# The low parts of the attention scores as two 64-row matmuls, one per half of the keys

## The chip, the cores and the metric

One core of one Trainium2 chip. The metric is the device time of one execution in microseconds (us), the median of several runs. PE is TensorE (matmuls; its weight loads are listed as PEld), DVE is VectorE, ACT is ScalarE, POOL is GpSimd, SP is SyncE, which issues nearly all DMAs.

## What is computed

Attention over 4 batches x 8 heads (32 heads here, sequence 576, head dimension 64) with an additive position bias, and two feed-forward layers behind it:

```python
scores = scale * np.matmul(q, k.transpose(0, 1, 3, 2)) + bias
attn = softmax(scores)                 # over the keys, denominator + 1e-9
x = np.matmul(attn, v)                 # heads side by side: 2304 tokens x 512
r = np.maximum(x @ w_in, 0.0)
x = (s * r * r + b) @ w_out            # 512 -> 2048 -> 512
h = x @ w_in2
out = (h - np.tanh(h)) @ w_out2        # 512 -> 2048 -> 512
```

The bias is the product of a two-layer network of log distances, one 576 x 576 map for each of the 8 heads.

## The kernel before

Products that need more than one matmul pass's precision are made from high and low parts: `x` is rounded to a shorter float (`high`), and `x - high` is `low`. q and k arrive from memory twice, stacked: partitions 0 to 63 and 64 to 127 hold the same 64 x 576 values (`q_raw`, `k_raw`). For q, ACT writes `q2 = round(q_raw * lower)` (L199), where `lower` is 0 in the upper 64 partitions and 1 in the lower ones, and POOL writes `q2 = q_raw - q2` (L209). So partitions 0 to 63 of `q2` hold q's high parts and 64 to 127 its low parts. For k, POOL writes `k2h = round(k_raw)` (L204) and `k2l = k_raw - k2h` (L213), both over all 128 partitions. One matmul of `q2` with `k2h` gives high*high + low*high, one with `k2l` gives high*low + low*low.

A head is five steps (t = 0 to 4, `NT` = 5) of 128 rows of scores each, the last padded. Step g = 5 n + t does on PE (`pe_step`): the scores of head n, tile t (`pe_score`, L576 to 582: two halves of 288 keys, each in a PSUM bank of its own, a matmul with `k2h` and one with `k2l` per half, 4 in all); the product of earlier probabilities with v (`pe_value`, L556 and 559, for heads 0 to 9; `pe_value_planes`, L541 and 544, from head 10 on); and for heads 0 to 9 the transposition of the probabilities (`pe_turn`, L592). DVE adds the bias and takes the minimum (L764), ACT does the exponential (L640). From head 10 on the probabilities are written as two 16-bit planes (ACT L628, DVE L743), turned by a DMA (SP L807), and POOL casts the high plane to `pth` (L686) for the value matmul L541 of the step after.

Order on the engines is the order of the program text; semaphores tie them together. POOL in a step (`pool_step`): at t = 0 the rounding and low part of k of the next head, then the cast for a value matmul (from head 12 on), at t = 1 the scaling of x (L714, every other head, heads 0 to 9) and q's low part of the next head, at t = 3 the parts of v. ACT rounds q of the next head at the end of its t = 1. SP (`sp_step`) issues in each step the next head's bias tile (L219), then a plane's turning; at t = 1 the load of v, at t = 2 that of k and at t = 4 that of q two heads ahead (L817 to 821). Each raw buffer is single: `load_q` waits for `q_lo_done`, `load_k` for `k_lo_done`.

Up to 70 us the position bias is built (`*_biases`; PE multiplies in four 32-column tiles side by side, L424). Then steps run alone (`STEPS_AT[:FIRST]`, 49 steps, until about 181 us). From there the 5 x 64 feed-forward blocks run (`pe_block`, 12 matmuls each, L903 to 905; their low weights come from POOL, L860, three blocks ahead, behind ACT's high weights, L853), and the other steps are put between them at the places of the list `PLACES`: behind every second block in parts, behind every block in others. Heads 10 and on lie there, until about 745 us.

`o_tmp` holds the lower half of a head's output for a moment (ACT L645 writes it, DVE L781 reads it).

Of the kernel before, what the change touches and what calls it, by code (L numbers as in the profile page):

```python
# [5 lines left out]
F32 = mybir.dt.float32  # L6
# [6 lines left out]
P = 128  # L13
# [18 lines left out]
def build(nc, qt, kt, vt, net, w2s, psi, lam, lam_rows, sb, w1, w2, w3, w4, out):  # L32
# [53 lines left out]
    with ExitStack() as ctx:  # L86
# [11 lines left out]
        v_raw = tile("v_raw", [P, 2 * NT - 1, D])  # L98
        q2 = tile("q2", [P, 2, NT * P], F32R)
        k2h = tile("k2h", [P, 2, S], F32R)  # L100
        k2l = tile("k2l", [P, 2, S], F32R)
        bias_t = tile("bias_t", [P, NT, S])

        zero_done = sem("zero_done")
# [21 lines left out]
        v_hi_done = sem("v_hi_done")  # L126
        q_lo_done = sem("q_lo_done")
        k_lo_done = sem("k_lo_done")
        v_lo_done = sem("v_lo_done")
        s_done = sem("s_done")  # L130
        min_done = sem("min_done")
# [74 lines left out]
        def pool_low_q(pool, n):  # L206
            pool.wait_ge(q_hi_done, n + 1)
            both = q2[:, n % 2, 0:S]
            pool.tensor_tensor(both, q_raw[:], both.bitcast(F32), ALU.subtract).then_inc(q_lo_done, 1)  # L209

        def pool_low_k(pool, n):
            pool.wait_ge(k_hi_done, n + 1)
            pool.tensor_tensor(k2l[:, n % 2, :], k_raw[:], k2h[:, n % 2, :].bitcast(F32), ALU.subtract)\  # L213
                .then_inc(k_lo_done, 1)

        def sp_bias(sp, n, t):
            R = ROWS[t]
# [6 lines left out]
        with nc.sbuf_tensor("ptl", [P, 2, S], F32R) as ptl:  # L224
            pass
        planes = tile("planes", [P, 2, 2 * S], F16)
        o_tmp = tile("o_tmp", [D, 2, HALF])
        neg_max = tile("neg_max", [P, NT])
        den = tile("den", [P, 2, NT])
        den_e = tile("den_e", [P, NT])  # L230
# [98 lines left out]
        def act_biases(act):  # L329
            act.dma_start(net_c, net).then_inc(net_loaded, DMA)  # L330
            act.dma_start(lam_c, lam).then_inc(psi_loaded, DMA)
            act.wait_ge(table_done, 2)

            def hidden(pack):
                need(act, hid_used, pack - HIDS + 1)
                n = reach(pack)
                for at in range(VEC, PACK):
                    step = pack * PACK + at
                    mm = act.activation(hid[:, pack % HIDS, at, 0:n], psi_w[:, 0:n], ACT.Relu,  # L339
                                        bias=knee[:, step:step + 1])  # L340
                mm.then_inc(hid_act, 1)

            hidden(0)
            act.wait_ge(table_done, 4)
            for pack in range(PACKS):
                if pack + 1 < PACKS:
                    hidden(pack + 1)
                back, ahead = backward(pack), forward(pack)
                act.wait_ge(hid_used, pack + 1)
                if pack >= RES_BUFS:  # L350
                    act.wait_ge(stage_stored[pack % RES_BUFS], pack // RES_BUFS * DMA)
                for acc, lo, hi in chunks(pack):
                    hi = min(hi, ahead)
                    if lo < hi:
                        dst = stage[:, pack % RES_BUFS, back + lo:back + hi]
                        mm = act.activation(dst, acc[:, 0:hi - lo], ACT.Copy,  # L356
                                            scale=row_scale[:, pack:pack + 1])
                mm.then_inc(ahead_done, 1)
                if pack == LATE:
                    act.wait_ge(q_clear, 2)  # L360
                    act.wait_ge(lower_done, 2)
                    act_round_q(act, 0)

        def pool_biases(pool):
            pool.memset(ident[:], 0.0).then_inc(zero_done, 1)
            pool.memset(bias_t[:, NT - 1, :], 0.0).then_inc(bias_clear, 1)
            for par in range(2):
                pool.memset(q2[:, par, S:NT * P].bitcast(F32), 0.0).then_inc(q_clear, 1)
            pool.wait_ge(zero_done, 1)
            pool.affine_select(out=ident[:], in_=ident[:], compare_op=ALU.not_equal, fill=1.0, base=0,  # L370
                               pattern=[[-1, P]], channel_multiplier=1).then_inc(ident_done, 1)
            pool_round_k(pool, 0)
            pool_low_k(pool, 0)
            pool_low_q(pool, 0)

        def dve_biases(dve):
# [145 lines left out]
        def cast(g):  # L522

            return g - NT - 2 if FIRST_PLANE <= g - NT - 2 < TILES else None
# [38 lines left out]
        def pe_score(pe, n, t):  # L563
            if t == 0:
                pe.wait_ge(q_lo_done, n + 1)
                pe.wait_ge(k_lo_done, n + 1)
            if n == 0:
                need(pe, min_done, t - 1)
                pe.wait_ge(back_done, PACKS - 2 if t == 0 else PACKS)
            elif n <= TURNED:  # L570
                pe.wait_ge(min_done, n * NT + t)
            else:
                if n == TURNED + 1 and t == 0:
                    pe.wait_ge(pt_lo_done, FIRST_PLANE)
                pe.wait_ge(p_lo_done, n * NT + t - FIRST_PLANE - 1)
            for half in range(2):  # L576
                cols = slice(half * HALF, (half + 1) * HALF)
                acc = score_bank(n, t)[:, half, 0:HALF]
                lhs = q2[:, n % 2, P * t:P * (t + 1)]
                pe.matmul(acc, lhs, k2h[:, n % 2, cols], start=True, stop=False)  # L580
                mm = pe.matmul(acc, lhs, k2l[:, n % 2, cols], start=False, stop=True)  # L581
            mm.then_inc(s_done, 1)

        def pe_turn(pe, i, alone):
# [46 lines left out]
        def act_step(act, g, alone, between=None):  # L631
            n, t = divmod(g, NT)
            i, j = turned(g), valued(g)

            def exponential():
                if t == 0:
                    need(act, den_done, min(n - 1, TURNED))
                act.wait_ge(min_done, g + 1)
                p = score_home(n, t)
                act.activation(p, p, ACT.Exp, scale=-1.0, bias=neg_max[:, t:t + 1],  # L640
                               accum_out=den[:, n % 2, t:t + 1]).then_inc(exp_done, 1)

            if j is not None and j % NT == NT - 1:
                act.wait_ge(pv_done, j + 1)
                act.activation(o_tmp[:], ps_o[D:P, :, 0:HALF], ACT.Copy, scale=1.0 if j < FIRST_PLANE else PLANE)\  # L645
                    .then_inc(o_low_done, 1)
            f = planes_of(g)
            if f is not None:
                act_plane(act, f)
            if scoring(n) and alone and t == NT - 1:  # L650
                exponential()
            if i is not None:
                R = ROWS[i % NT]
                act.wait_ge(pt_done, i + 1)
                need(act, pv_done, i - 1)
                act.activation(pth[0:R, slot(i), :], turn_bank(i, alone)[0:R, 0:S], ACT.Copy)\
                    .then_inc(pt_hi_done, 1)
            if n < TURNED and between:
                between()
            if scoring(n) and not (alone and t == NT - 1):  # L660
                exponential()
            if n >= TURNED and between:
                between()
            if TURNED <= n < BH:
                act.wait_ge(exp_done, g + 1)
                act.activation(sum_n[:, t:t + 1], den[:, n % 2, t:t + 1], ACT.Copy, scale=PLANE, bias=1e-9 * PLANE)\
                    .then_inc(sum_done, 1)
            if t == 0 and turning(n):
                v = n - 1
                need(act, inv_done, v)  # L670
                act.wait_ge(exp_done, (v + 1) * NT)
                act.activation(den_e[:], den[:, v % 2, :], ACT.Copy, bias=1e-9).then_inc(den_done, 1)
            if t == 1 and n + 1 < BH:
                act_round_q(act, n + 1)

        def pool_step(pool, g):
            n, t = divmod(g, NT)
            if t == 0 and n + 1 < BH:
                pool_round_k(pool, n + 1)
                pool_low_k(pool, n + 1)  # L680
            i = cast(g)
            if i is not None:
                if i % NT == 0:
# [63 lines left out]
        def dve_step(dve, g, alone, between=None):  # L747
# [29 lines left out]
            if j is not None and j % NT == NT - 1:  # L777
                h = j // NT
                dve.wait_ge(o_low_done, h + 1)
                dst = x_slice(h, slice(h % 2 * D, (h % 2 + 1) * D))  # L780
                dve.scalar_tensor_tensor(out=halves(dst), in0=ps_o[0:D, :, 0:HALF],  # L781
                                         scalar=1.0 if h < TURNED else PLANE, in1=o_tmp[:],
                                         op0=ALU.mult, op1=ALU.add).then_inc(o_done, 1)
            if between:
                between()
# [1 line left out]
        def sp_step(sp, g):  # L787
# [29 lines left out]
                load_v(sp, n)  # L817
            if t == 2 and n + 2 < BH:
                load_k(sp, n + 2)
            if t == 4 and n + 2 < BH:  # L820
                load_q(sp, n + 2)

        def raw_block(b):
# [230 lines left out]
        def _(pe):  # L1054
            pe_biases(pe)
            pe.wait_ge(ident_done, 1)
            pe.wait_ge(q_clear, 2)
            for g in STEPS_AT[:FIRST]:
                pe_step(pe, g, True)
            pe.wait_ge(pt_lo_done, turned(FIRST - 1))  # L1060
# [68 lines left out]
```

## Time and profile before

| | |
|---|---|
| median of 3 runs | 1100.48 us (1098.94 to 1100.62) |
| profiled execution, its own time | 1100.58 us |
| its span from first to last instruction | 1098.8 us |
| granted TensorE clock, mean | 0.995 |
| PE busy | 1050.3 us (96%), 5668 matmuls |
| DVE, ACT, POOL busy | 617.6 us, 732.3 us, 680.9 us |

Durations in the profile are of single instructions. Matmuls are pipelined: one is listed as 0.29 to 0.38 us long, while the next may start 0.13 or 0.21 us after it, so what PE's stream costs is read from start to start. A time in square brackets behind an instruction is how long its engine sat idle before it and what released it.

### The profile page before, as it was taken

To read this page: it belongs to the slowest core of one execution; us is meant where nothing else is said; L and a number is where in the kernel's file an instruction comes from. 1 tells how busy PE (TensorE), PEld (TensorE's weight loads), DVE (VectorE), ACT (ScalarE), POOL (GpSimd) and SP (SyncE) were. 2 spreads that over 40 slices of the span, in tenths; PEclk is the share of its full clock that TensorE was granted. 3 is DMA by queue.
4 is the path that set the end of the run, shared out by engine and by line. 5 is a ranking of instruction groups with operands and counts; after the bars stand their busy time and mean duration, and the time that the engine had idled before them with its cause. 6 is when DMAs were issued, how large, how long until landed. Compare 5 with 4: busy or idle time off the path is not lost.

```text
span 1098.8 us, 16840 instructions
## 1 busy us (share of the span) xinstructions
PE 1050.3 (96%) x5668; PEld 912.9 (83%) x5668; DVE 617.6 (56%) x1120; ACT 732.3 (67%) x1477; POOL 680.9 (62%) x656
## 2 busy tenths in 40 slices
PE   4669999999999999999999999999999999999998
PEld 1148889888888888888888888888888888999998
DVE  5968877745775476468646754771350451440640
ACT  8968887866877687678767776873562563553652
POOL 1046675677778677777786777765554555455453
PEclk9989999999999999999999999999999999999999
DMA  4678876799779778987896799764323233332331
GB/s 166 242 247 260 278 228 173 190 245 239 193 213 263 211 196 216 258 216 203 237 275 167 193 256 263 174 161 130 112 98 115 96 107 131 106 129 101 97 122 64
DMA packets 185482, 202.51 MB, mean 184 GB/s; under 512 B 125954, under 2 KB 128692, under 8 KB 185396
## 3 DMA queue, kind: packets, MB, share of 16 engines
q1 hardware_dynamic: 185108, 201.35, 65.5%
q8 instruction: 46, 0.75, 0.3%
q14 instruction: 40, 0.33, 0.1%
q10 hardware_dynamic: 288, 0.07, 0.0%
HBM read 156.55 MB, written 15.64 MB: 157 GB/s over the span
## 4 chain that ended last, share of the span: by engine, by line
PE 71%; ACT 11%; issue 7%; POOL 5%; DVE 4%; DMA 2%; SPq 0%; DVEq 0%; ACTq 0%; POOLq 0%
PE ps_f L903 20%; PE ps_f L905 20%; PE ps_f L904 20%; ACT x_raw L339 3%; POOL wl L860 2%; PE ps_o L541 2%; DVE g_buf L963 2%; PE ps_s L580 2%; PE ps_s L581 2%; ACT gh L916 2%; PE ps_o L544 2%; ACT stage L356 2%; PE ps_o L556 1%; POOL pth L686 1%; ACT planes L628 1%
## 5 line engine op out<-in xcount | busy, mean ns | idle before, releaser
L860 POOL TENSOR_TENSOR wl<-w_raw,wh 128x512 fp32r<-128x512 f32 x318 | 417.0, 1317 | 285.2 <-ACT wh L853 284.7
L903 PE MATMUL ps_f<-gh,wh 128*128 128x464 f32 (+1 forms) x640 | 243.3, 380 | 1.6 <-DVE g_buf L963 1.6
L903 PE MATMUL ps_f<-xh,wh 128*128 128x464 f32 (+1 forms) x640 | 240.6, 376 | 0.6 <-DVE ptl L732 0.6
L904 PE MATMUL ps_f<-gl,wh 128*128 128x464 f32 (+1 forms) x640 | 238.1, 372 | 0.0
L905 PE MATMUL ps_f<-gh,wl 128*128 128x464 f32 (+1 forms) x640 | 237.9, 372 | 0.0
L905 PE MATMUL ps_f<-xh,wl 128*128 128x464 f32 (+1 forms) x640 | 237.5, 371 | 0.0
L904 PE MATMUL ps_f<-xl,wh 128*128 128x464 f32 (+1 forms) x640 | 237.2, 371 | 0.0
L853 ACT ACTIVATE wh<-w_raw 128x512 fp32r<-128x512 f32 x318 | 196.4, 623 | 49.1 <-PE ps_f L905 48.6
L903 PEld LDWEIGHTS ps_f<-gh,wh 128*128 128x128 f32 x640 | 121.3, 190 | 14.9 <-DVE g_buf L963 2.8
L903 PEld LDWEIGHTS ps_f<-xh,wh 128*128 128x128 f32 x640 | 120.5, 188 | 13.3 <-DVE ptl L732 0.8
L905 PEld LDWEIGHTS ps_f<-gh,wl 128*128 128x128 f32 x640 | 120.6, 188 | 13.0
L905 PEld LDWEIGHTS ps_f<-xh,wl 128*128 128x128 f32 x640 | 120.2, 188 | 13.4
L904 PEld LDWEIGHTS ps_f<-xl,wh 128*128 128x128 f32 x640 | 120.2, 188 | 12.7
L904 PEld LDWEIGHTS ps_f<-gl,wh 128*128 128x128 f32 x640 | 120.7, 189 | 11.8
L926 ACT ACTIVATE r_buf<-ps_f 128x464 f32<-128x464 f32 (+1 forms) x160 | 87.9, 550 | 59.2 <-PE ps_f L905 58.3
L954 DVE TENSOR_TENSOR gl<-g_buf,gh 128x464 fp32r<-128x464 f32 (+1 forms) x80 | 81.3, 1016 | 47.5 <-ACT gh L920 47.5
L951 DVE SCALAR_TENSOR_TENSOR gl<-g_buf,sb_c,gh 128x464 fp32r<-128x464 f32 (+1 forms) x80 | 73.9, 924 | 52.9 <-ACT gh L916 52.9
L963 DVE SCALAR_TENSOR_TENSOR g_buf<-ps_f,sb_c,r_buf 128x464 f32<-128x464 f32 (+1 forms) x80 | 55.4, 693 | 41.6 <-ACT r_buf L926 40.2
L686 POOL CAST pth<-p_t 128x576 fp32r<-128x576 f16 x110 | 77.5, 704 | 0.0
L209 POOL TENSOR_TENSOR q<-q_raw,q 128x576 fp32r<-128x576 f32 x32 | 45.9, 1434 | 46.1 <-ACT q L199 46.1
L580 PE MATMUL ps_s<-k2h,q 128*128 128x288 f32 x210 | 65.4, 326 | 5.7 <-DVE neg_max L764 5.7
L916 ACT ACTIVATE gh<-g_buf,sb_c 128x464 fp32r<-128x464 f32 (+1 forms) x80 | 54.3, 678 | 20.9 <-DVE g_buf L963 20.9
(124 smaller groups left out, 1693.0 us busy)
## 6 DMA issues: line engine op xcount, KB each, us to landing
w_raw<-in_w_out SPq DMA_DIRECT2D x80, 512.0 KB, 3.6
w_raw<-in_w_in SPq DMA_DIRECT2D x79, 512.0 KB, 3.5
bias_t<-bias_flat SPq DMA_DIRECT2D x128, 288.0 KB, 4.0
bias_flat<-stage SPq DMA_DIRECT2D x36, 295.5 KB, 2.2
k_raw<-in_kt SPq DMA_DIRECT2D x32, 288.0 KB, 4.0
q_raw<-in_qt SPq DMA_DIRECT2D x32, 288.0 KB, 3.3
v_raw<-in_vt SPq DMA_DIRECT2D x32, 288.0 KB, 3.2
bias_t<-bias_flat SPq DMA_DIRECT2D x32, 144.0 KB, 4.1
```

What stands on the lines that cost most here:

```text
L580: pe.matmul(acc, lhs, k2h[:, n % 2, cols], start=True, stop=False)
L686: pool.tensor_copy(pth[:, slot(i), :], turned_planes(i // NT)[:, i % NT, :]).then_inc(block_cast, 1)
L853: act.activation(wh[:, b % RING, :, :], raw_block(b), ACT.Copy)\
L860: pool.tensor_tensor(wl[:, b % RING, :, :], raw_block(b), wh[:, b % RING, :, :].bitcast(F32), ALU.subtract).then_inc(w_lo_done, 1)
L903: pe.matmul(acc, hi, rhs_h[:, k0 + kk, 0:T], start=(first and kk == 0), stop=False)
L904: pe.matmul(acc, hi, rhs_l[:, k0 + kk, 0:T], start=False, stop=False)
L905: mm = pe.matmul(acc, lo, rhs_h[:, k0 + kk, 0:T], start=False, stop=(last and kk == 3))
L916: act.activation(gh[:, j, 0:T], g_buf[:, n % 2, 0:T], ACT.Identity, bias=sb_c[:, 1:2])\
L926: act.activation(r_buf[:, n % 2, 0:T], acc, (ACT.Relu, ACT.Tanh)[l]).then_inc(r_done, 1)
L951: dve.scalar_tensor_tensor(out=gl[:, j, 0:T], in0=g_buf[:, n % 2, 0:T], scalar=sb_c[:, 1:2], in1=hi, op0=ALU.add, op1=ALU.subtract).then_i ...
L954: dve.tensor_tensor(gl[:, j, 0:T], g_buf[:, n % 2, 0:T], hi, ALU.subtract)\
L963: dve.scalar_tensor_tensor(out=g_buf[:, n % 2, 0:T], in0=acc, scalar=sb_c[:, 0:1], in1=r, op0=ALU.mult, op1=ALU.mult).then_inc(g_done, 1)
```

## The change

`k2l` keeps for each half of the partitions only one half of the keys: partitions 0 to 63 hold k's low parts for keys 0 to 287, 64 to 127 those for keys 288 to 575. POOL writes it with two subtractions of 64 partitions x 288, the second after the first has ended. q's high parts are needed in the lower partitions too: POOL copies `q_raw` there into a new tile with rounding (`q_even`, `q_odd` by head), at t = 0 behind k's low part, and goes on when the copy has ended. In `pe_score` the two matmuls with `k2h` come first, then two of 64 rows: q's high parts from partitions 0 to 63 with the left half of k's low parts into the first bank, and from partitions 64 to 127 with the right half into the second. The product of the two low parts is no longer computed. `o_tmp` uses partitions 0 to 63 of the place where `q_even` uses 64 to 127. The load of q is issued at t = 3 in place of t = 4.

```diff
-        k2l = tile("k2l", [P, 2, S], F32R)
+        k2l = tile("k2l", [P, 2, HALF], F32R)
+        q_odd = tile("q_odd", [P, NT * P], F32R)
+        with nc.sbuf_tensor("o_tmp", [P, 2, HALF], F32) as o_tmp:
+            pass
+        q_even = tile("q_even", [P, NT * P], F32R)
...
         def pool_low_k(pool, n):
             pool.wait_ge(k_hi_done, n + 1)
-            pool.tensor_tensor(k2l[:, n % 2, :], k_raw[:], k2h[:, n % 2, :].bitcast(F32), ALU.subtract)\
-                .then_inc(k_lo_done, 1)
+            pool.tensor_tensor(k2l[0:D, n % 2, :], k_raw[0:D, 0:HALF], k2h[0:D, n % 2, 0:HALF].bitcast(F32),
+                               ALU.subtract).then_inc(k_left_done, 1)
+            pool.wait_ge(k_left_done, n + 1)
+            pool.tensor_tensor(k2l[D:P, n % 2, :], k_raw[D:P, HALF:S], k2h[D:P, n % 2, HALF:S].bitcast(F32),
+                               ALU.subtract).then_inc(k_lo_done, 1)
+
+        def q_below(n):
+
+            return q_odd if n % 2 else q_even
+
+        def pool_round_q(pool, n):
+            pool.wait_ge(q_loaded, (n + 1) * DMA)
+            pool.wait_ge(k_lo_done, n + 1)
+            pool.tensor_copy(q_below(n)[D:P, 0:S], q_raw[D:P, :]).then_inc(q_below_done, 1)
+            pool.wait_ge(q_below_done, n + 1)
...
             for par in range(2):
                 pool.memset(q2[:, par, S:NT * P].bitcast(F32), 0.0).then_inc(q_clear, 1)
+                pool.memset(q_below(par)[:, S:NT * P].bitcast(F32), 0.0).then_inc(q_clear, 1)
...
             pool_round_k(pool, 0)
             pool_low_k(pool, 0)
+            pool_round_q(pool, 0)
             pool_low_q(pool, 0)
...
                 pe.matmul(acc, lhs, k2h[:, n % 2, cols], start=True, stop=False)
-                mm = pe.matmul(acc, lhs, k2l[:, n % 2, cols], start=False, stop=True)
+            for half, high in ((0, q2[0:D, n % 2, P * t:P * (t + 1)]), (1, q_below(n)[D:P, P * t:P * (t + 1)])):
+                acc = score_bank(n, t)[:, half, 0:HALF]
+                mm = pe.matmul(acc, high, k2l[half * D:(half + 1) * D, n % 2, :], start=False, stop=True)
             mm.then_inc(s_done, 1)
...
             if t == 0 and n + 1 < BH:
                 pool_round_k(pool, n + 1)
                 pool_low_k(pool, n + 1)
+                pool_round_q(pool, n + 1)
...
-            if t == 4 and n + 2 < BH:
+            if t == 3 and n + 2 < BH:
                 load_q(sp, n + 2)
```

## Rows read from the trace of the kernel before

**Rows 1.** Busy time by stretch: stretch, its length, busy us of each engine (instructions), clock.

```profile
70.00:181.00 111.00, 103.93 (x681) 92.81 (x682) 87.09 (x184) 90.29 (x193) 69.31 (x69) 0.97 0.78 244
181.00:745.00 564.00, 556.65 (x2916) 490.45 (x2915) 356.33 (x665) 413.65 (x867) 418.34 (x426) 1.00 0.85 217
```

**Rows 2.** PE in order of time, mixed stretch: start us, duration us, engine, line, operation.

```profile
400.35 0.37 PE L905 MATMUL ps_f<-xh,wl 128*128 128x464 f32 x1
400.56 0.30 PE L580 MATMUL ps_t<-k2h,q 128*128 128x288 f32 x1
400.69 0.29 PE L581 MATMUL ps_t<-k2l,q 128*128 128x288 f32 x1
```

**Rows 3.** The matmuls and weight loads of L581 alone, by stretch.

```profile
70.00:181.00 111.00, 27.10 (x94) 18.63 (x94) 0.97 0.78 244
181.00:745.00 564.00, 60.18 (x216) 40.59 (x216) 1.00 0.85 217
```

**Rows 4.** PE and its loads in order of time, full array to 64 columns.

```profile
129.92 0.29 PE L559 MATMUL ps_o<-ptl,vhl 128*128 128x288 f32 x1
...
129.93 0.57 PEld L592 LDWEIGHTS ps_t<-ident,p_t 128*64 128x64 f32 x5
...
130.05 0.71 PE L592 MATMUL ps_t<-ident,p_t 128*64 128x128 f32 x5
```

**Rows 5.** PE in order of time where 32-column tiles end and scores begin.

```profile
61.85 1.18 PE L424 MATMUL ps_o<-x_raw,y 128*32 128x288 f32 x16 [0.37 <-ACT x_raw L339]
...
62.58 0.45 PE L424 MATMUL ps_o<-x_raw,y 128*32 128x288 f32 x4
...
62.96 0.40 PE L580 MATMUL ps_s<-k2h,q 128*128 128x288 f32 x1
63.20 0.30 PE L581 MATMUL ps_s<-k2l,q 128*128 128x288 f32 x1
```

**Rows 6.** POOL by line, 181 to 745 us: shapes, count | busy us, mean ns | idle before.

```profile
L860 POOL TENSOR_TENSOR wl<-w_raw,wh 128x512 fp32r<-128x512 f32 x173 | 228.3, 1322 | 115.0 <-ACT wh L853 114.7
...
L213 POOL TENSOR_TENSOR k2l<-k_raw,k2h 128x576 fp32r<-128x576 f32 x20 | 29.0, 1450 | 1.6
L705 POOL TENSOR_TENSOR vhl<-v_raw,vhl 128x320 fp32r<-128x320 f32 x22 | 20.5, 932 | 0.0
```

**Rows 7.** POOL and PE in order of time at a head's first step.

```profile
332.00 0.67 POOL L204 CAST k2h<-k_raw 128x576 fp32r<-128x576 f32 x1
...
332.75 1.41 POOL L213 TENSOR_TENSOR k2l<-k_raw,k2h 128x576 fp32r<-128x576 f32 x1
...
334.12 1.07 POOL L686 CAST pth<-p_t 128x576 fp32r<-128x576 f16 x1
...
335.24 0.40 PE L541 MATMUL ps_o<-pth,vhl 128*128 128x288 f32 x1 [1.55 <-POOL pth L686]
```

**Rows 8.** The same cast and its matmul at two other heads' first steps.

```profile
352.44 0.67 POOL L686 CAST pth<-p_t 128x576 fp32r<-128x576 f16 x1
...
353.34 0.30 PE L541 MATMUL ps_o<-pth,vhl 128*128 128x288 f32 x1
...
387.19 1.08 POOL L686 CAST pth<-p_t 128x576 fp32r<-128x576 f16 x1
...
389.13 0.29 PE L541 MATMUL ps_o<-pth,vhl 128*128 128x288 f32 x1
```

**Rows 9.** A lone step in order of time: the minimum and the score behind it.

```profile
108.89 0.73 DVE L764 CUSTOM_DVE_ANT_0 p_t<-ps_s,bias_t 128x576 f32<-128x576 f32 x1
...
109.69 0.40 PE L580 MATMUL ps_s<-k2h,q 128*128 128x288 f32 x1
```

**Rows 10.** POOL's idle time in the lone stretch, and the landing of q's loads (L184).

```profile
108.60 1.43 POOL L209 TENSOR_TENSOR q<-q_raw,q 128x576 fp32r<-128x576 f32 x1 [1.91 <-ACT q L199]
...
117.76 1.42 POOL L714 TENSOR_TENSOR x_raw<-x_raw,inv_b 128x576 f32<-128x576 f32 x1 [2.81 <-DMA inv_b<-inv_rows]
...
DMA to landing us min/median/max: 2.8/3.3/6.0
```

More of the change, by code:

```diff
@@ L128, in build @@
         k_lo_done = sem("k_lo_done")
+        k_left_done = sem("k_left_done")
+        q_below_done = sem("q_below_done")
         v_lo_done = sem("v_lo_done")
@@ L226, in build @@
         planes = tile("planes", [P, 2, 2 * S], F16)
-        o_tmp = tile("o_tmp", [D, 2, HALF])
         neg_max = tile("neg_max", [P, NT])
@@ L359, in act_biases @@
                 if pack == LATE:
-                    act.wait_ge(q_clear, 2)
+                    act.wait_ge(q_clear, 4)
                     act.wait_ge(lower_done, 2)
@@ L644, in act_step @@
                 act.wait_ge(pv_done, j + 1)
-                act.activation(o_tmp[:], ps_o[D:P, :, 0:HALF], ACT.Copy, scale=1.0 if j < FIRST_PLANE else PLANE)\
+                act.activation(o_tmp[0:D, :, :], ps_o[D:P, :, 0:HALF], ACT.Copy, scale=1.0 if j < FIRST_PLANE else PLANE)\
                     .then_inc(o_low_done, 1)
@@ L781, in dve_step @@
                 dve.scalar_tensor_tensor(out=halves(dst), in0=ps_o[0:D, :, 0:HALF],
-                                         scalar=1.0 if h < TURNED else PLANE, in1=o_tmp[:],
+                                         scalar=1.0 if h < TURNED else PLANE, in1=o_tmp[0:D, :, :],
                                          op0=ALU.mult, op1=ALU.add).then_inc(o_done, 1)
@@ L1056, in _ @@
             pe.wait_ge(ident_done, 1)
-            pe.wait_ge(q_clear, 2)
+            pe.wait_ge(q_clear, 4)
             for g in STEPS_AT[:FIRST]:
```

## The prediction

> **What bounds the kernel now.** I read the busy time by stretch first. From 70 to 181 us the steps run alone, from 181 to 745 us between the blocks of the feed-forward part; before lies the building of the bias, behind it the blocks by themselves, and the change touches neither. In the two stretches PE is busy 94 and 99% of the time [rows 1]. Modelled ends make PE look busier than it is, so I then read start to start in the list in order of time [rows 2]: a block's matmul of 464 columns starts 0.21 us before the next one, a score matmul of 288 columns 0.13 us. Only few gaps are longer, so PE's stream is the path from 70 us to the end, and 0.1 us more or less in each step shows in the total. Inside a lone step there is a second loop: there is one score bank, so the minimum on DVE (L764) releases the score [rows 9], and the score releases the next minimum.
>
> The other thing to see is who else stops PE. Between 181 and 745 us the value matmul L541 waits for the POOL cast L686, 1.55 us in the case shown [rows 7]. All such long waits lie at the first step of a head, where POOL does k's rounding and k's low part ahead of the cast. POOL is busy only 74% of that stretch [rows 1], but it works its queue in order.
>
> **PE, the pair.** Before, a step's scores are four matmuls, 4 x 0.13 = 0.52 us, two of them with the low part of k. These two (0.26 us) become two 64-row matmuls in different rows of the array and different PSUM banks. If they run truly side by side the pair costs one matmul and a start, some 0.14 us: 0.12 us saved. Each still has its own weight load of 128 columns. No row shows a 64-row load; the nearest is a chain of five loads in 0.57 us where the last is 0.11 long, (0.57 - 0.11)/4 = 0.115 us apart [rows 4]. If the two loads go one after the other, the pair costs 0.23 us: 0.03 us saved. I take the middle, 0.08 us, and keep 0.03 and 0.12 as ends. There are 216/2 = 108 steps with scores in the mixed stretch and 94/2 = 47 in the lone one [rows 3]. Mixed: 108 x 0.08 = 8.6 us (3.2 to 13.0). Lone: the score lies on both loops, but at a head's end PE waits for other things, so I count 40 of 47: 3.2 us (1.2 to 4.8).
>
> **PE, the change of tiling.** Each step now goes from full matmuls to 64-row ones and back. What does this cost? The kernel before already changes shape, by columns: L592 with 64 columns follows L559 at the usual 0.13 us, its weights being loaded 0.01 us after L559 starts, so nothing is drained and the load stays hidden [rows 4]. A change from 32-column tiles to the full array is there once: the 16 matmuls of L424 go four side by side from 61.85, the last four from 62.58, so a wave takes (62.58 - 61.85)/3 = 0.24 us and the last is through at 62.82. L580 starts at 62.96 and its successor 0.24 instead of 0.13 us later [rows 5]. That is up to 0.14 + 0.11 = 0.25 us, but L580 may have waited for a semaphore there. So a switch costs 0 to 0.25 us; I take 0, by the nine 64-column cases, of which one is shown [rows 4], since they are met in the running stream. The Trainium skill, "TensorEngine Tiling (Array Packing)", Key Properties, says that changing the tiling mode drains the TensorE. For columns the trace doesn't agree (0.13 us across the change); for rows nothing here shows it, and the first rival is that rule.
>
> **POOL, the head's start.** In the first step of each head (L213 replaced) POOL did k2h, k2l and then the cast; the cast started 1.37 us behind k2l's start [rows 7]. Now k2l is two instructions of 288 columns, each waiting for the one before, and q's rounding (576 columns into the lower half) comes on top, also with waits on both sides. From 1450 ns for 576 and 932 ns for 320 columns [rows 6] a column costs 2.0 ns, so a half takes 0.83 us from the 1.41 shown [rows 7], 0.87 from the mean, and 0.71 if there is no fixed part at all. The copy is of k2h's kind and length, 0.67 us, and a dependent successor starts 0.08 us after its end [rows 7]. 2 x 0.83 + 0.67 + 3 x 0.08 = 2.57 us, less 1.37: 1.2 us more (0.95 to 1.27). That partitions are halved saves nothing where the columns stay; the trace has no POOL row at 64 partitions, and this is a choice.
>
> Who waits for it? In the mixed stretch 19 first steps both prepare a next head and cast. I took for each the time from the cast's end to its matmul. In five it is 0.05 us: PE is already waiting [rows 7]. In two it is 0.23 and in three 0.45, in seven 0.85 or 0.86, and in two 3.3 us; one of the 0.23 and one of the 0.86 are shown [rows 8]. Seventeen are so short that 1.2 us goes through. The added wait is 17 x 1.2 - (5 x 0.05 + 2 x 0.23 + 3 x 0.45 + 7 x 0.85) = 20.4 - 8.0 = 12.4 us (8.1 to 13.6). In these heads PE also arrives a step's gain earlier and loses it again, 17 x 0.08 = 1.4 us. The long casts, 1.07 instead of 0.67 us [rows 7, 8], show POOL held up while DVE works; more POOL instructions can meet this more often, which I leave in the range. Later POOL work of a head is covered: POOL then waits for wh anyway (115 us in sum [rows 6]) and catches up.
>
> In the lone stretch the same 1.2 us is hidden. POOL idles behind k2l: 2.8 us until inv_b lands in heads that scale x, about 1.9 us until ACT has rounded q in the others [rows 10]. The copy needs q_raw, which ACT's rounding waits for too, and takes 0.67 us where ACT takes 0.78. Without that cover 1.2 us x 9 heads = 11 us would come.
>
> **The rest costs nothing.** load_q moves on SP from t 4 to t 3, behind that step's bias load and waiting for q_lo_done, which POOL gives at t 1 or early in t 3; queued behind it are the next bias load and, mixed, a plane's transposition, and it is done some 1 us before the next is due. It lands in 3.3 us, at most 6.0 [rows 10], about two steps before POOL needs it. Left at t 4, the copy would wait. Two more small memsets lie at the very start, far ahead of the first score at 62.96 us [rows 5]. o_tmp only moves. The order high, high, low, low keeps the number of matmuls, and the semaphore still sits on the last one.
>
> **The sum.** The profiled execution took 1100.58 us (span 1098.8 and 1.8 around it), 0.1 from the median 1100.48. -8.6 - 3.2 + 1.4 + 12.4 = +2.0: 1102.6 us. With the ends: 0.12 saved and 0.95 added gives -13.0 - 4.8 + 2.0 + 8.1 = -7.7, 1093; 0.03 and 1.27 gives -3.2 - 1.2 + 0.5 + 13.6 = +9.7, 1110.
>
> **The rivals.** (1) The switch costs. If each of two exposes a weight load (0.11 us, as behind L580 there, 0.24 for 0.13 [rows 5]), a step loses 0.22 - 0.08 = 0.14: 108 x 0.14 + 40 x 0.14 = 21 us, and PE being slower hides some of POOL's line (9 us left): 1130. If only one of them pays it is 3 + 1 + 12: 1117. With 0.25 each: 0.42 x 148 = 62, POOL 3: 1166. For it: no row shows a 64-row tile between full ones. Against it: the change by columns that costs nothing [rows 4]. (2) Faster: POOL's longer line doesn't reach PE. POOL idles 115 us waiting for wh [rows 6], so the chain could start from something that has play, and halves on 64 partitions may be quicker than I priced. It decides if the added line is under the 0.05 to 0.85 us of play, that is below about 0.3 us. Then only PE's gain is left, 12 to 18 us: 1083 to 1089. Against it: the five places where PE already waits have no play. (3) The two matmuls don't overlap at all, so the change doesn't do what it says: no gain, POOL's 12.4 us stay: 1113.
>
> **How the numbers follow.** A difference under 0.2%, 2.2 us, can't be told from none. Forecast 0.48 (1093 to 1110: of it faster 0.13, same 0.17, slower 0.18), rival 1 0.27, rival 2 0.20, rival 3 0.05. Faster 0.13 + 0.20 = 0.33, same 0.17, slower 0.18 + 0.27 + 0.05 = 0.50. The range goes from 1087, inside rival 2, to 1134, above rival 1's 1130, and leaves out its upper part and a little of rival 2. The forecast's own range is 1093 to 1110.
>
> **What would show it.** The two 64-row matmuls starting 0.01 to 0.1 us apart, the first full matmul behind them at 0.14 to 0.23 us from the pair's start: the gain is right. A start 0.3 us or more behind, with its weight load not begun before: rival 1. Waits of L541 for L686 growing by about 12 us, at head starts, cast 1.2 us later behind k2h: POOL's term is right; if they stay as they are, rival 2. In the lone stretch POOL's q low part must start right behind ACT's rounding as before. The prediction is wrong if a switch has a price, or if ACT (90 of 111 us busy in the lone stretch [rows 1]) or DVE takes over as PE gets quicker.

## The result and the profile after

The changed kernel takes 1132.8 us (1132.0 to 1133.5), the kernel before 1100.5: the ratio is 1.0293, with a 95% interval of 1.0280 to 1.0307. It is slower by 32.3 us.

First the stream of PE, one mixed step in order of time. L600 is the matmul with `k2h`, L603 one of the two with 64 rows, L561 and L564 the value matmuls, L926 the next block:

```profile
416.52 0.37 PE L928 MATMUL ps_f<-xh,wl 128*128 128x464 f32 x1
416.73 0.43 PE L600 MATMUL ps_t<-k2h,q 128*128 128x288 f32 x2
417.09 0.40 PE L603 MATMUL ps_t<-k2l,q 64*128 64x288 f32 x1
417.09 0.40 PE L603 MATMUL ps_t<-k2l,q_even 64*128 64x288 f32 x1
417.42 0.40 PE L561 MATMUL ps_o<-pth,vhl 128*128 128x288 f32 x1
417.65 0.30 PE L564 MATMUL ps_o<-p_t 128*128 128x288 f16 x1
...
417.96 0.47 PE L926 MATMUL ps_f<-xh,wh 128*128 128x464 f32 x1
```

The kernel before in the same kind of step, from its last score matmul on ([rows 2] show its start, at 400.56), with the weight load of the first value matmul:

```profile
400.95 0.29 PE L581 MATMUL ps_t<-k2l,q 128*128 128x288 f32 x1
400.95 0.19 PEld L541 LDWEIGHTS ps_o<-pth,vhl 128*128 128x128 f32 x1
401.08 0.29 PE L541 MATMUL ps_o<-pth,vhl 128*128 128x288 f32 x1
401.22 0.30 PE L544 MATMUL ps_o<-p_t 128*128 128x288 f16 x1
...
401.53 0.47 PE L903 MATMUL ps_f<-xh,wh 128*128 128x464 f32 x1
```

The pair does start together (417.09 twice), so it costs one matmul and not two. But it starts 0.36 us after the first of the two full matmuls, which take 2 x 0.13 = 0.26 in a running stream; the next full matmul starts 0.33 us after the pair in place of 0.13; and the one behind that (L564) starts 0.23 us after L561, before it was 0.14. 0.10 + 0.20 + 0.10 is lost, 0.13 gained: from the first score matmul to the next block 417.96 - 416.73 = 1.23 us, before 401.53 - 400.56 = 0.97.

The weight loads of the same stretch show where it goes:

```profile
416.52 0.40 PEld L600 LDWEIGHTS ps_t<-k2h,q 128*128 128x128 f32 x2
417.08 0.18 PEld L603 LDWEIGHTS ps_t<-k2l,q 64*128 64x128 f32 x1 [0.17 <-issue]
417.09 0.18 PEld L603 LDWEIGHTS ps_t<-k2l,q_even 64*128 64x128 f32 x1
417.41 0.19 PEld L561 LDWEIGHTS ps_o<-pth,vhl 128*128 128x128 f32 x1
```

The first load of L600 starts with the matmul before it (416.52), ahead of its own at 416.73: that is how a load is hidden. The pair's loads start only at 417.08, with their matmuls, and L561's load at 417.41, with its own. At both changes the load is in the open. What it waited for the profile doesn't name (`issue`); that the matmuls in front had to run out first is my reading of it.

Then POOL and PE at a head's first step, where rows 7 show the same head before:

```profile
342.69 0.67 POOL L210 CAST k2h<-k_raw 128x576 fp32r<-128x576 f32 x1
343.44 0.80 POOL L219 TENSOR_TENSOR k2l<-k_raw,k2h 64x288 fp32r<-64x288 f32 x1
344.32 1.07 POOL L222 TENSOR_TENSOR k2l<-k_raw,k2h 64x288 fp32r<-64x288 f32 x1
345.53 0.66 POOL L232 CAST q_odd<-q_raw 64x576 fp32r<-64x576 f32 x1
346.25 0.67 POOL L709 CAST pth<-p_t 128x576 fp32r<-128x576 f16 x1
...
346.97 0.61 PE L561 MATMUL ps_o<-pth,vhl 128*128 128x288 f32 x1 [2.26 <-POOL pth L709]
```

From the start of k's low part to the cast it is 2.81 us here, and 1.37 before; over the 19 heads the mean is 2.69 against 1.37. PE's wait in front of the value matmul is 2.26 us here where it was 1.55.

To split the loss I summed, in each kernel, the time from the first score matmul of a step behind a block to the first matmul of the next block; there are 110 such steps. "Above the median" is what these sums hold above 110 times the median, which is waiting (the median is read to 0.01 us, so this column is good to about 1 us). The next column is the start of the first such step, which holds what the lone steps cost. In the kernel before the first block starts at 158.1 us, and not at about 181 as said further up: 49 steps lie ahead of it, and 110 directly behind a block, where the prediction counted 47 and 108. All columns but the last are read from the one traced execution of each kernel.

| kernel | median step | sum of 110 | above the median | first mixed step at | time |
|---|---|---|---|---|---|
| before | 0.97 | 117.0 | 10.3 | 163.2 | 1100.5 |
| after | 1.24 | 147.3 | 10.9 | 168.3 | 1132.8 |
| pair_only | 1.24 | 140.2 | 3.8 | 167.3 | 1123.9 |
| pool_only | 0.98 | 132.6 | 24.8 | 165.2 | 1114.9 |
| same_rows | 1.37 | 153.1 | 2.4 | 172.8 | 1142.7 |
| apart | 1.75 | 195.2 | 2.7 | 188.3 | 1200.3 |
| narrow | 0.97 | 117.2 | 10.5 | 167.1 | 1100.9 |
| after_cast_first | 1.24 | 138.4 | 2.0 | 167.3 | 1122.8 |
| before_cast_first | 0.97 | 112.7 | 6.0 | 162.9 | 1097.4 |

For the changed kernel: 30.3 us in these steps and 5.1 in the part ahead of them, while all that lies between and behind takes 3.1 us less, in part since they no longer wait for DVE (the page has 1.6 us of waits of L903 for g_buf before and none after): 32.3 us, which is also the difference of the two spans (1131.1 and 1098.8).

The column of the first mixed step needs care. In narrow it is 3.9 us later than before although the kernel is no slower: its traced execution had a span of 1102.8 us, and the median of its ten executions is 1100.9. In that trace PE waits for q's low part from POOL, 0.87 us at 104.36 and 1.06 us at 143.79, where POOL had waited 3.94 and 4.32 us for `inv_b` to land (3.25 in the first of the two heads before); between most other scores the lone steps take what they took before. In pair_only the delay is even instead: from the 11th score on, ten lone steps take 19.6 us each time, before 18.8 to 19.0. That is the kernel's own.

### The profile page after: what moved, and what is told of

It reads as the page before. It is cut to its first block, busy times and chain, and to the rows that moved or that the text cites. A ratio compares the mean times of both kernels' runs of the same rounds, so it can differ in the third digit from the quotient of the medians.

```text
span 1131.1 us, 16970 instructions
## 1 busy us (share of the span) xinstructions
PE 1083.4 (96%) x5668; PEld 905.0 (80%) x5668; DVE 619.2 (55%) x1120; ACT 736.5 (65%) x1477; POOL 708.6 (63%) x722
## 4 chain that ended last, share of the span: by engine, by line
PE 72%; POOL 14%; issue 6%; ACT 5%; DMA 2%; DVE 0%; SPq 0%; POOLq 0%; ACTq 0%; DVEq 0%
PE ps_f L928 19%; PE ps_f L926 19%; PE ps_f L927 19%; POOL wl L883 6%; PE ps_o L561 3%; ACT x_raw L357 3%; POOL pth L709 3%; PE ps_s L603 2%; PE ps_s L600 2%; PE ps_o L576 2%; ACT stage L374 1%; POOL k2l L222 1%; PE ps_t L614 1%; PE ps_o L564 1%; POOL k2l L219 1%
## 5 line engine op out<-in xcount | busy, mean ns | idle before, releaser
L926 PE MATMUL ps_f<-gh,wh 128*128 128x464 f32 (+1 forms) x640 | 242.9, 380 | 0.0
L926 PE MATMUL ps_f<-xh,wh 128*128 128x464 f32 (+1 forms) x640 | 240.7, 376 | 0.8 <-DVE ptl L755 0.4
L926 PEld LDWEIGHTS ps_f<-xh,wh 128*128 128x128 f32 x640 | 120.5, 188 | 14.0 <-POOL xl L745 0.7
L926 PEld LDWEIGHTS ps_f<-gh,wh 128*128 128x128 f32 x640 | 121.2, 189 | 12.0
L561 PE MATMUL ps_o<-pth,vhl 128*128 128x288 f32 x220 | 70.1, 383 | 9.6 <-POOL pth L709 8.7
```

The source lines that it names most:

```text
L561: mm = pe.matmul(ps_o[:, half, 0:HALF], vhl[:, n % 2, u, :], pth[:, slot(i), cols], start=(u == 0), stop=(u == NT - 1))
L926: pe.matmul(acc, hi, rhs_h[:, k0 + kk, 0:T], start=(first and kk == 0), stop=False)
```

## The experiments

Two theories stood: the change of tiling by rows costs time at each switch (rival 1 of the prediction), or POOL's longer line at a head's start does it, which the sum of the prediction had as its largest loss. The first four runs take one part of the change each.

**pair_only.** The pair on PE, all else as before.

```diff
-                mm = pe.matmul(acc, lhs, k2l[:, n % 2, cols], start=False, stop=True)
+            for half in range(2):
+                rows, cols = slice(half * D, (half + 1) * D), slice(half * HALF, (half + 1) * HALF)
+                acc = score_bank(n, t)[:, half, 0:HALF]
+                mm = pe.matmul(acc, q2[rows, n % 2, P * t:P * (t + 1)], k2l[rows, n % 2, cols], start=False, stop=True)
```

> The 64-row pair of the changed kernel on PE, everything else as before: POOL's one subtraction of 576 columns, no copy of q, load of q at t = 4. The second matmul of the pair takes the rows 64 to 127 of q2, which hold q's low parts, so low*low stands where high*low belongs in the right half; the work is the same. Theory 1 (the two switches of tiling carry the whole loss, 0.27 us a mixed step): 1128 to 1133, like the changed kernel. Theory 2 (POOL's longer line at a head's start carries about 12 us of the 32, as the forecast's sum had it): 1119 to 1122.

Measured: 1123.9 us, ratio 1.0211 (1.0196 to 1.0226). PE's part alone costs 23.3 us. Neither number fits: 9 us are missing to the changed kernel, so POOL's work does cost something there, but less than 12. The median step is 0.27 us longer, as in the changed kernel (29.7 us in 110 steps); the waits shrink from 10.3 to 3.8 us, as a slower PE comes later to a cast that is as late as before.

**pool_only.** POOL and q's load as in the changed kernel, PE as before.

```diff
-            pool.tensor_tensor(k2l[:, n % 2, :], k_raw[:], k2h[:, n % 2, :].bitcast(F32), ALU.subtract)\
-                .then_inc(k_lo_done, 1)
+            pool.tensor_tensor(k2l[:, n % 2, 0:HALF], k_raw[:, 0:HALF], k2h[:, n % 2, 0:HALF].bitcast(F32),
+                               ALU.subtract).then_inc(k_left_done, 1)
+            pool.wait_ge(k_left_done, n + 1)
+            pool.tensor_tensor(k2l[:, n % 2, HALF:S], k_raw[:, HALF:S], k2h[:, n % 2, HALF:S].bitcast(F32),
+                               ALU.subtract).then_inc(k_lo_done, 1)
...
+            pool.tensor_copy(q_copy[D:P, 0:S], q_raw[D:P, :]).then_inc(q_below_done, 1)
+            pool.wait_ge(q_below_done, n + 1)
...
-            if t == 4 and n + 2 < BH:
+            if t == 3 and n + 2 < BH:
```

> PE as before, POOL as in the changed kernel: the subtraction for k in two parts of 288 columns (over all partitions), the rounded copy of q into the lower partitions (which nobody reads), their waits, and q's load at t = 3. This measures the forecast's POOL term by itself. The forecast's term says +12 us (8 to 14): 1109 to 1114. If POOL's line has play that the forecast missed: 1100 to 1104.

Measured: 1114.9 us, ratio 1.0129 (1.0114 to 1.0144), 14.3 us more. The median step is unchanged and the waits grow from 10.3 to 24.8 us. So the price of POOL's line (12.4 forecast, 8.1 to 13.6) was a little low on a PE that is otherwise as before. The two parts by themselves make 23.3 + 14.3 = 37.6 us, together 32.3: they overlap by 5 us.

**same_rows.** Two 64-row matmuls, but both in rows 0 to 63, so that they run one after the other.

```diff
-                mm = pe.matmul(acc, lhs, k2l[:, n % 2, cols], start=False, stop=True)
+            for half in range(2):
+                cols = slice(half * HALF, (half + 1) * HALF)
+                acc = score_bank(n, t)[:, half, 0:HALF]
+                mm = pe.matmul(acc, q2[0:D, n % 2, P * t:P * (t + 1)], k2l[0:D, n % 2, cols], start=False, stop=True)
```

> Both low matmuls have 64 rows, but both take the rows 0 to 63, so they can't run side by side; POOL as before, no copy of q. Two switches of tiling in a step, as in the pair. If the pair gains one matmul (0.13 us) by running side by side and a switch costs 0.20: a mixed step is 0.40 longer than before, 110 steps 44 us, the lone ones a few more: 1145 to 1152. If the loss came from the pair itself (two loads or two banks at a time) and not from the switch: below the pair's time, 1100 to 1115.

Measured: 1142.7 us, ratio 1.0382 (1.0366 to 1.0397). The step is 1.37 us, 0.40 above before, as expected; the total is a little under the expectation because the other waits nearly vanish (2.4 us). In order of time on PE, with the two weight loads of L584:

```profile
415.68 0.37 PE L908 MATMUL ps_f<-xh,wl 128*128 128x464 f32 x1
415.89 0.43 PE L580 MATMUL ps_s<-k2h,q 128*128 128x288 f32 x2
416.25 0.53 PE L584 MATMUL ps_s<-k2l,q 64*128 64x288 f32 x2
416.25 0.29 PEld L584 LDWEIGHTS ps_s<-k2l,q 64*128 64x128 f32 x2 [0.17 <-issue]
416.71 0.40 PE L541 MATMUL ps_o<-pth,vhl 128*128 128x288 f32 x1
```

The two of L584 run from 416.25 and the next full one starts 0.46 us later; the pair side by side leaves 0.33. So side by side is worth 0.13 us, one whole matmul, and a change in and one out cost 0.40. The two loads are 0.18 to 0.19 us long and end together at 416.54, so the second starts at 416.36, ahead of its matmul at 416.49: between two matmuls of the same 64 rows the load is hidden again.

**order_only.** The kernel before with its four full matmuls in the new order (both with `k2h`, then both with `k2l`).

> The kernel before with its four full score matmuls in the order of the changed kernel: both with k2h, then both with k2l. If order plays no part, as theory 1 has it: 1100.5 within 1 us. If closing both banks at the end delays DVE or the next loads: 1103 or more.

Measured: 1100.7 us, ratio 1.0002 (0.9993 to 1.0012). The order plays no part.

**apart.** The changed kernel with each 64-row matmul behind its own full one.

```diff
             for half in range(2):
...
                 pe.matmul(acc, lhs, k2h[:, n % 2, cols], start=True, stop=False)
-            for half, high in ((0, q2[0:D, n % 2, P * t:P * (t + 1)]), (1, q_below(n)[D:P, P * t:P * (t + 1)])):
-                acc = score_bank(n, t)[:, half, 0:HALF]
+                high = (q2[0:D, n % 2, P * t:P * (t + 1)], q_below(n)[D:P, P * t:P * (t + 1)])[half]
```

> The changed kernel with the two 64-row matmuls apart: high of half 0, its 64-row matmul, high of half 1, its 64-row matmul. Four switches in a step, nothing side by side. Theory 1, from the starts in the pair's trace (0.23 us into the pair, 0.32 out, and 0.10 on the next load): a step is 0.68 to 0.80 us longer than before in place of 0.27, 1170 to 1190. If a switch costs only once in a step, whatever the number (the next load queue, say): 1140 to 1150.

Measured: 1200.3 us, ratio 1.091 (1.0894 to 1.0927), above the expected span. The step in order of time:

```profile
433.24 0.37 PE L927 MATMUL ps_f<-xh,wl 128*128 128x464 f32 x1
433.45 0.29 PE L600 MATMUL ps_s<-k2h,q 128*128 128x288 f32 x1
433.68 0.40 PE L602 MATMUL ps_s<-k2l,q 64*128 64x288 f32 x1
434.00 0.40 PE L600 MATMUL ps_s<-k2h,q 128*128 128x288 f32 x1
434.33 0.40 PE L602 MATMUL ps_s<-k2l,q_even 64*128 64x288 f32 x1
434.66 0.40 PE L561 MATMUL ps_o<-pth,vhl 128*128 128x288 f32 x1
```

Between two changes a matmul takes 0.32 to 0.33 us in place of 0.13: 0.20 us for each change, whichever way it goes. Where the load before the first change was still hidden (L600 at 433.45) its matmul takes 0.23, 0.10 more than in a running stream; where its own load is in the open too, 0.20 more. I read the first 0.10 as the running out and the second as the open load; the price of the change doesn't hang on this split. The median step is 1.75 us, 0.78 above before, four times 0.195: the price is per switch and adds up. The step is where it was expected; the total lies above because the 49 lone steps lose 25 us, for which the expectation had hardly counted anything.

**narrow.** A change of tiling by columns in the same place: the two matmuls with `k2l` get 64 columns of q as weights. The low part of the lower half of each score tile is left out.

```diff
-                pe.matmul(acc, lhs, k2h[:, n % 2, cols], start=True, stop=False)
-                mm = pe.matmul(acc, lhs, k2l[:, n % 2, cols], start=False, stop=True)
+                pe.matmul(acc, lhs, k2h[:, n % 2, cols], start=True, stop=True)
+            for half in range(2):
+                cols = slice(half * HALF, (half + 1) * HALF)
+                acc = score_bank(n, t)[0:D, half, 0:HALF]
+                lhs = q2[:, n % 2, P * t:P * t + D]
+                mm = pe.matmul(acc, lhs, k2l[:, n % 2, cols], start=False, stop=True, skip_group_check=True)
```

> A change of tiling by columns in the running stream: the kernel before, but the two matmuls with k2l have only the first 64 columns of q2 as weights (tile 128 x 64 in place of 128 x 128), behind the two with k2h, so there is one change in and one out per step. The low part of the rows 64 to 127 of each score tile is left out. All 128 rows of the array work. As the 64-column transpositions of before suggested, a change by columns costs nothing: 1099 to 1102. If every change of tiling drains, as by rows: like two 64-row matmuls in the same rows, 1140 to 1145.

Measured: 1100.9 us, ratio 1.0008 (0.9999 to 1.0017). This change by columns, 128 to 64 and back, costs nothing that can be told from none, and its loads stay hidden:

```profile
404.48 0.43 PE L580 MATMUL ps_t<-k2h,q 128*128 128x288 f32 x2
404.62 0.27 PEld L585 LDWEIGHTS ps_t<-k2l,q 128*64 128x64 f32 x2
404.75 0.43 PE L585 MATMUL ps_t<-k2l,q 128*64 128x288 f32 x2
404.88 0.19 PEld L541 LDWEIGHTS ps_o<-pth,vhl 128*128 128x128 f32 x1
405.02 0.29 PE L541 MATMUL ps_o<-pth,vhl 128*128 128x288 f32 x1
```

The loads at 404.62 and 404.88 lie 0.13 us ahead of their matmuls at 404.75 and 405.02, across both changes, where in the pair they start with them. The Trainium skill, "TensorEngine Tiling (Array Packing)", Key Properties, says of all changes of tiling mode that they drain the TensorE. The runs agree with it for rows (0.20 us a change), and not for this change by columns (none).

**after_cast_first and before_cast_first.** In a head's first step POOL does the cast ahead of the work on k (and q).

```diff
-            if t == 0 and n + 1 < BH:
-                pool_round_k(pool, n + 1)
-                pool_low_k(pool, n + 1)
             i = cast(g)
             if i is not None:
...
                 pool.tensor_copy(pth[:, slot(i), :], turned_planes(i // NT)[:, i % NT, :]).then_inc(block_cast, 1)
+            if t == 0 and n + 1 < BH:
+                pool_round_k(pool, n + 1)
+                pool_low_k(pool, n + 1)
```

This is the kernel before; in the changed one `pool_round_q` moves with them.

> The changed kernel, but in a head's first step POOL does the cast for the value matmul before it rounds k, forms its low parts and copies q. This takes POOL's longer line off the path and leaves its work. If the rest of the loss beyond the pair on PE (1132.8 - 1123.9 = 9 us) is this line: 1122 to 1125, with waits for the cast down to a few us. If it is POOL's amount of work or the earlier load of q: 1130 to 1133.

> The same order on POOL in the kernel before. PE and its loads wait there up to 12 us for casts, most of it at heads' first steps: if these waits go, 1092 to 1096, which would beat both kernels. If something else is due at the same places (DVE and ACT are close behind in the first quarter of each unit): 1097 to 1100.

Measured: the changed kernel falls to 1122.8 us, ratio 1.0209 to the kernel before (1.0195 to 1.0223), so POOL's line carried 10 of its 32 us, and what is left is the pair's. The kernel before falls to 1097.4 us, ratio 0.9978 (0.9969 to 0.9987): faster than both, though by only 2.5 us: the second case of the expectation, and not the 4 to 8 us of the first. Who waited for the cast, in the trace of the kernel before, in the changed one, and in the latter with the cast first (total us, times), shows that the waits went:

```profile
  PEld ps_o L541: 7.3, 8
  PE ps_o L541: 4.6, 3
```

```profile
  PEld ps_o L561: 14.1, 20
  PE ps_o L561: 8.7, 10
```

```profile
  PEld ps_o L561: 3.3, 5
  PE ps_o L561: 1.7, 2
```

Loads and matmuls wait at the same time, so the two lines of one kernel aren't added. In the kernel before the steps' sum falls by 4.3 us with the cast first, and the span of the traced execution by 4.0 (1098.8 to 1094.8). That the medians lie only 2.5 us apart is a matter of which executions were traced: that of the kernel before was 0.7 us above the 1099.9 that it had as median in this comparison, the other 0.8 below its own. What the 6.0 us of waits are that stay is open.

**pool_only_cast_first.** pool_only with the cast first.

> The kernel with the changed kernel's POOL work and PE as before (1114.9), but with the cast for the value matmul ahead of the work on k and q in a head's first step. If the 14 us are the line ahead of the cast and not POOL's amount of work: 1097 to 1100, near the kernel before with its cast first (1097.4). If the amount counts: 1105 to 1112.

Measured: 1098.1 us, ratio 0.998 (0.9968 to 0.9992). All of the 14.3 us are gone with the order alone, and the 2.5 that it gives the kernel before come on top: it was the line ahead of the cast and not the amount of POOL's work.

**after_load_t4.** The changed kernel with q's load at t = 4, as before.

```diff
-            if t == 3 and n + 2 < BH:
+            if t == 4 and n + 2 < BH:
                 load_q(sp, n + 2)
```

> The changed kernel with q's load left at t = 4. The forecast said that POOL's copy of q would then wait for the load at a head's first step, and the cast behind it. Where blocks and steps alternate one to one, the load would be issued some 3.6 us before the copy and lands in 3 to 6: a wait of 1 to 2 us at about every second head, 1138 to 1150. If the load has play there: 1132 to 1134.

Measured: 1140.0 us, ratio 1.0353 (1.0328 to 1.0378) to the kernel before, 7 us above the changed kernel. POOL's copy waits for the load in 11 cases, 11.4 us in sum; one of them, with q's load issued on SP in the line above it:

```profile
366.61 0.58 SPq L190 DMA_DIRECT2D q_raw<-in_qt  x1
...
367.79 0.81 POOL L222 TENSOR_TENSOR k2l<-k_raw,k2h 64x288 fp32r<-64x288 f32 x1
370.01 0.66 POOL L232 CAST q_even<-q_raw 64x576 fp32r<-64x576 f32 x1 [1.41 <-DMA q_raw<-in_qt]
```

The load is issued at 366.61 and the copy can start at 370.01. The earlier load is a needed part of the change.

## Why the prediction came out as it did

The forecast, 1102.6 us, was too low by 30 us; slower was its likelier side, and the time lies within the range only at its upper end, which was put there for rival 1 and its 1130. The forecast's own range, 1093 to 1110, misses it. By its steps:

- **The pair side by side: right in kind, too small in size.** 0.08 us was taken, 0.12 was the upper end; it is 0.13 (same_rows against pair_only, 1.37 - 1.24). The two loads of the pair, which I had feared to follow one another, start 0.01 us apart.
- **The change of tiling at nothing: this step failed.** It is the term that carries the miss: 0 in the sum, 0.40 us a step in the runs. "I take 0, by the nine 64-column cases" carried a price from changes by columns to a change by rows. narrow shows that these cases were read rightly and apart that they say nothing on rows: 0.20 us for each change. The other row, of the transition from 32-column tiles [rows 5], was nearer in size (0 to 0.25), and narrow suggests that it was a wait and not the change of tiling after all; that is not shown, since those were tiles at other columns.
- **Rival 1: right in kind, half the size.** It had an exposed load of 0.11 us for each change; the runs show 0.20. Its sum (a step loses 0.14, POOL 9 us left, 1130) lands near 1132.8 partly because errors cancel: the step loses 0.27, which is 30 us in the mixed part, 14 us more than it had. Against that, 6.5 us of the waits that PE had before vanish behind the slower PE (10.3 to 3.8 in pair_only), and what lies between and behind the steps takes 3.1 us less. That 1130 is so near is in part luck.
- **Lone steps: over-counted.** I counted 40 of 47 steps with the full price. pair_only starts its first mixed step 4.0 us later, 0.08 us for each of 49 steps. There the load at a score's start and behind a transposition was in the open before too, as in the 0.24 us behind L580 [rows 5], and in the lone step of [rows 9], where L580 and its load both start at 109.69 and L581 0.24 us later; so one of the prices was paid already. In apart it is 25 us, 0.51 a step.
- **POOL's line: right, a little low.** Half a subtraction takes 0.80 us in the median (0.83 forecast) with 64 partitions, and 0.81 with 128 (pool_only), so halving them saves nothing; the line is 1.32 us longer in the mean (1.2 forecast), 1.17 in nine heads and 1.46 in ten where an instruction is held up; alone it costs 14.3 us (12.4 forecast). That a slower PE hides part of it was right too (9 us left forecast; 8.9 against pair_only, 10.0 with the cast first).
- **Rival 2** fell with pool_only, **rival 3** with the pair's starts. q's load at t 3 was needed, as the prediction said, and POOL's work in the lone stretch cost little: pool_only begins its first mixed step 2 us later, which is less than the 3.9 us of narrow, whose time is that of the kernel before.

## What to carry to other kernels

Two 64-row matmuls side by side save one matmul (here 0.13 us), but each change between 64 and 128 rows in a running stream costs 0.20 us, so a block of 64-row work has to hold more than three such pairs in a row before it gains (an estimate, 0.40 / 0.13; no run has more than one pair in a row). A price read from one kind of change, here tiling by columns, doesn't hold for another; where no row shows the thing itself, give the written rule against it more than a quarter. And before work is added to an in-order queue, put what another engine waits for ahead of it: here that order alone is worth 17 us to the added work by itself (1114.9 to 1098.1), 10 in the changed kernel, and 2.5 without any.

## What the runs showed of the hardware that I hadn't expected

- A change of the number of rows, 128 to 64 or back, costs 0.20 us in these runs (apart: four changes, 0.78 us), and at it the weight load doesn't start ahead of its matmul. A change of the number of columns, 128 to 64 and back, costs nothing (ratio 1.0008), and its loads go ahead as usual.
- Two loads and two matmuls in different halves of the rows start within 0.01 us of each other, so a pair takes no longer than one; of two in the same rows the second load is hidden (416.36, its matmul 416.49).
- POOL's time goes by columns and not by partitions: 0.80 us for 64 x 288, 0.81 for 128 x 288 (pool_only), 1.43 for 128 x 576 (medians); 0.66 for a rounding copy of 64 x 576 where 128 x 576 takes 0.67.
